# Attention units of one pair of heads over half a batch instead of over a whole batch, with the scores negated, in a fused attention and two-layer feed-forward kernel

## The reference

```python
q_d, k_d, v_d = mean of q, k, v over groups of 4 tokens        # 144 pooled tokens
out_up = repeat(softmax_attention(q_d, k_d, v_d), 4)
mask = |pos_i - pos_j| < 4
out_local = softmax(where(mask, scale * q k^T, -1e9)) v        # softmax subtracts the maximum, adds 1e-9 to the sum
x = (out_up + out_local), heads side by side                   # 2304 x 512
h = relu(x @ w_in); g = s * h * h + b; x = g @ w_out           # d_ff 2048
out = ((x @ w_a) * (x @ w_b)) @ w_out2                         # d_ff 1536
```

## Time and profile before

| | us |
|---|---|
| median of 3 runs | 1069.96 (1068.77 to 1071.46) |
| the profiled execution, whole | 1069.81 |
| its span in the trace | 1068.0 |
| PE busy in the span | 1009.2 (94%) |
| DVE, ACT, POOL busy | 442.6, 356.3, 159.4 |
| start of the first matmul of slot 0 and of slot 1 of the first layer | 74.10, 81.21 |
| start of the second layer | 596.06 |

### The profile page before, as it was taken

How to read it: one execution, slowest core, us unless ns; L and a number is a source line. 1 busy time by engine, 2 the same in 40 slices (tenths; PEclk the granted TensorE clock), 3 DMA queues, 4 the chain that set the end, 5 groups by cost and what they waited for, 6 DMA issues and landing times.

```text
span 1068.0 us, 17004 instructions
## 1 busy us (share of the span) xinstructions
PE 1009.2 (94%) x6984; PEld 944.7 (88%) x6984; DVE 442.6 (41%) x800; ACT 356.3 (33%) x791; POOL 159.4 (15%) x126
## 2 busy tenths in 40 slices
PE   5678899999999999999999799999999999999997
PEld 4557889999999999999999699899899898998996
DVE  4768665565555655554345521211211212112111
ACT  3445444444344443344245421211211212212211
POOL 4545343122331223310000000000000000000000
PEclk9659999999999999999999899999999999999999
DMA  7343401121011210201033600010100100100000
GB/s 193 77 124 112 126 20 50 45 68 46 17 52 46 68 46 15 55 13 43 10 111 119 200 1 1 20 40 1 57 3 1 60 1 1 60 1 1 30 2 30
DMA packets 98829, 52.50 MB, mean 49 GB/s; under 512 B 60384, under 2 KB 92768, under 8 KB 98752
## 3 DMA queue, kind: packets, MB, share of 16 engines
q1 hardware_dynamic: 98608, 51.35, 17.3%
q10 hardware_dynamic: 144, 0.07, 0.0%
HBM read 41.97 MB, written 9.44 MB: 48 GB/s over the span
## 4 chain that ended last, share of the span: by engine, by line
PE 85%; DVE 6%; ACT 3%; POOL 3%; issue 2%; DMA 1%; SPq 0%; ACTq 0%; DVEq 0%; POOLq 0%
PE bank L667 28%; PE bank L632 18%; PE bank L617 17%; PE bank L681 13%; PE bank L546 2%; PE bank L493 2%; PE bank L517 2%; PE bank L467 1%; DVE relu L992 1%; POOL sm L1073 1%; PE bank L478 1%; POOL sm L1081 1%; PE bank L538 1%; POOL wx L1088 1%; PE bank L512 1%
## 5 line engine op out<-in xcount | busy, mean ns | idle before, releaser
L667 PE MATMUL bank<-x_hi,wx 128*128 128x384 f32 x1152 | 307.0, 337 | 11.8 <-DVE prod L1051 7.8
L632 PE MATMUL bank<-g_hi,wx 128*128 128x288 f32 x1024 | 234.2, 305 | 1.4 <-DVE o_sb L1004 1.4
L617 PE MATMUL bank<-wx 128*128 128x288 f32 x1536 | 230.7, 299 | 0.4 <-ACT relu L792 0.4
L667 PEld LDWEIGHTS bank<-x_hi,wx 128*128 128x128 f32 x1152 | 210.2, 188 | 17.3 <-issue 14.4
L617 PEld LDWEIGHTS bank<-wx 128*128 128x128 f32 x1536 | 211.8, 190 | 3.4 <-issue 2.8
L667 PE MATMUL bank<-x_lo,wx 128*128 128x384 f32 x576 | 193.5, 336 | 0.0
L632 PEld LDWEIGHTS bank<-g_hi,wx 128*128 128x128 f32 x1024 | 171.9, 189 | 9.5 <-issue 4.2
L1051 DVE TENSOR_TENSOR prod<-bank,a_sb 128x384 f32<-128x384 f32 x72 | 40.1, 558 | 314.5 <-ACT a_sb L854 314.5
L632 PE MATMUL bank<-g_lo,wx 128*128 128x288 f32 x512 | 151.5, 296 | 0.0
L992 DVE SCALAR_TENSOR_TENSOR relu<-relu,s_col 128x288 f32<-128x288 f32 x128 | 81.7, 638 | 166.4 <-ACT relu L792 166.2
L854 ACT ACTIVATE a_sb<-bank 128x384 f32<-128x384 f32 x72 | 35.3, 491 | 303.7 <-PE bank L667 303.7
(11 more groups left out here) (67 smaller groups left out, 821.4 us busy)
## 6 DMA issues: line engine op xcount, KB each, us to landing
nat<-in_q SPq DMA_DIRECT2D x32, 144.0 KB, 2.9
nat<-in_k SPq DMA_DIRECT2D x32, 144.0 KB, 3.2
vnat<-in_v SPq DMA_DIRECT2D x32, 144.0 KB
o_transposed<-o_sb SPq DMA_DIRECT2D x8, 576.0 KB, 3.2
o_raw<-o_transposed SPq DMA_DIRECT2D x6, 768.0 KB, 4.7
out<-y SPq DMA_DIRECT2D x18, 256.0 KB, 2.2
vwin<-in_v SPq DMA_DIRECT2D x32, 120.0 KB
raw<-in_moe_w_a SPq DMA_DIRECT2D x12, 256.0 KB, 3.1
```

The costliest lines, as they stand in the source:

```text
L617: mm = nc.tensor.matmul(HB[:, 0:HALF], wi(w, kd, f), xs(x, c % 2)[:, kd], start=(kd == 0 and j == 0), stop=(kd == KD - 1 and j == 2))
L632: mm = nc.tensor.matmul(ACC[o][:, 0:HALF], wo(w, f, o), g[:, slot % GB, :], start=(f == 0 and j == 0), stop=(f == F1 - 1 and j == 2))
L667: mm = nc.tensor.matmul(dst[:, 0:CH2], wab(w, f, j * KD + kd), x[:, kd, :], start=(kd == 0 and m == 0), stop=(kd == KD - 1 and m == 2))
```

## The change

The work is no longer cut by pair-batches but by units: one pair of heads over half a batch (288 tokens), 32 in all, in the order of the chunks of the first layer. A unit takes 4 slots. What needs the whole batch, which is k (turned and pooled) and the pooled v, is made by the unit of the first half of a batch (`leads(u)`) and kept for the second half. The boot now holds four units (first half of batch 0), each with a set of buffers of its own, and 28 units run beside the first layer. Within a unit:

- q and k are turned in ticks -5 and -4, that is in the gap between the scores and the turned probabilities of the unit before;
- pooled and local scores come together in tick 0, in banks 0, 1 and 2; the pooled and local probabilities are turned together in tick 6, the values come together in tick 7;
- q is scaled by -1/8, so scores have the other sign; the mask is subtracted, minima take the place of maxima, and the minimum goes into exp as a bias (scale -1). GpSimd's `subtract` goes; exp of the local scores is six instructions of 102 columns in place of one of 612;
- the 1e-9 is a column of the array that is summed, so one small addition goes;
- the pooled values are scaled by ScalarE (`take_up`, tick 8) and the sum of both (`take_values`, tick 8) is one VectorE instruction for each unit; `xf` has two buffers;
- 4 blocks of the first layer are split in the boot instead of 6, and from the seventh block on the second layer's are split behind each of its first six steps, none ahead of `take_acc`.

The first loads of k and q are shared by two DMA queues.

```diff
-POOLED, LOCAL0, LOCAL1 = 0, 1, 2
-JOBS = 3
-NP = PAIRS * B
-BOOT_SKEW = 6
-BOOT_END = 11
-BOOT_TICKS = BOOT_SKEW * (PAIRS - 1) + BOOT_END + 1
-BOOT_BLOCK_TICKS = (10, 14, 18, 22, 25, 28)
+NU = PAIRS * NCH
+SETS = PAIRS
+PER_UNIT = 2 * F1 // PAIRS
+LEAD = 3
+BOOT_SKEW = 6
+BOOT_TICKS = 34
+BOOT_BLOCK_TICKS = (-14, -9, -5, -3)
+EARLY2 = 6
...
+        def bank_before(u):
+
+            return max(u - 1, 0) if u <= PAIRS else u
+
+        def at_tick(g, boot_tick, tick):
+
+
+            first = [u for u in range(PAIRS) if BOOT_SKEW * u - BOOT_TICKS + boot_tick == g]
+            return first + [u for u in range(PAIRS, NU) if PER_UNIT * (u - PAIRS) - LEAD + tick == g]
...
+            def scores(u):
+                _, h, p = place(u)
+                at = base(u)
+                pe.wait_ge(kp_ready, pair(u) + 1)
+                pe.wait_ge(qp_ready, u + 1)
+                past(pe, ptl_taken, bank_before(u))
+                past(pe, o_taken, bank_before(u))
...
+                pooled_scores(0).then_inc(sp_half, 1)
+                for w in range(GW):
+                    for e in (1, 0):
+                        mm = local_scores(e, w)
+                mm.then_inc(sl_ready, 1)
+                pe.wait_ge(sp_half, u + 1)
+                pooled_scores(1).then_inc(sp_ready, 1)
...
+            def attention(g):
+                for u in at_tick(g, 12, 7):
+                    values(u)
+                for u in at_tick(g, 0, -5):
+                    if leads(u):
+                        turn_k(u)
+                for u in at_tick(g, 1, -4):
+                    turn_q(u)
+                for u in at_tick(g, 3, 0):
+                    scores(u)
+                for u in at_tick(g, 11, 6):
+                    turn_pooled(u)
+                for u in at_tick(g, 10, 6):
+                    turn_local(u)
...
+            def exp_local(u):
+                act.wait_ge(mnl_ready, u + 1)
+                for j in range(2 * GW):
+                    x = kits[kit(u)]["sml"][:, j, 0:WK]
+                    done = nc.scalar.activation(x, x, ACT.Exp, bias=mnl(u)[:, j:j + 1], scale=-1.0)
+                done.then_inc(el_ready, 1)
...
+            def take_up(u):
+                act.wait_ge(o_ready, u + 1)
+                past(act, o_taken, before(u))
+                nc.scalar.activation(kits[kit(u)]["up"][:], bank[:, base(u) + 2, HALF:HALF + GH], ACT.Copy,
+                                     scale=1.0 / POOL).then_inc(up_taken, 1)
...
             for slot in range(SLOTS):
                 c, f = divmod(slot, F1)
-                n, at = PAIRS + slot // 8, 2 * (slot % 8)
-                attention(n, at)
-                if slot % (2 * F1) in (1, 2, 3, 4):
-                    split_x_hi(c + 1, f - 1)
+                attention(2 * slot)
                 if f == 2 and c > 0:
                     take_acc(c - 1)
                 take_relu(slot)
-                attention(n, at + 1)
+                attention(2 * slot + 1)
...
-            for f in range(6, 9):
-                split_w2_hi(f)
             take_acc(NCH - 1)
...
+            def take_values(u):
+                dve.wait_ge(up_taken, u + 1)
+                past(dve, x_hi, u - 1)
+                past(dve, x_lo, u - 1)
+                dst = xf[:, u % 2, :].rearrange("p (g r) -> p g r", r=POOL)
+                src = bank[:, base(u) + 2, 0:HALF].rearrange("p (g r) -> p g r", r=POOL)
+                add = kits[kit(u)]["up"][:].unsqueeze(2).to_broadcast([P, GH, POOL])
+                nc.vector.tensor_tensor(dst, src, add, ALU.add).then_inc(o_taken, 1)
...
+            def attention(g):
+                for u in at_tick(g, 14, 8):
+                    take_values(u)
+                for u in at_tick(g, 15, 9):
+                    split_x_lo(u)
...
+                for u in at_tick(g, 4, 0):
+                    minima(u)
...
-            def subtract(n, kind):
-                pool.wait_ge(mx_ready, job(n, kind))
-                x = sm_flat(n, kind).rearrange("p (j c) -> p j c", c=WK)
-                m = mx(n, kind).unsqueeze(2).to_broadcast([WQ, 2 * GW, WK])
-                nc.gpsimd.tensor_tensor(x, x, m, ALU.subtract).then_inc(sub_ready, 1)
```

More of the change, by code:

```diff
@@ L306, in pt_bank, with place, leads, pair @@
-        def pt_bank(n):
-            return 4 * kit(n) + 2 if alone(n) else 1
-        def o_bank(n, kind):
-            return 4 * kit(n) + (1 if kind == LOCAL0 else 0) if alone(n) else 0
-        def boot_tick(at, tick_of):
-            return [p for p in range(PAIRS) if at - BOOT_SKEW * p == tick_of]
+        def place(u):
+            return u // (2 * PAIRS), u // PAIRS % 2, u % PAIRS
+        def leads(u):
+            return place(u)[1] == 0
+        def pair(u):
+            i, _, p = place(u)
+            return PAIRS * i + p
@@ L457, in _ @@
         def _(pe):
-            def turn(n, t):
-                if t == 0:
-                    pe.wait_ge(nat_in[kit(n)], 64 * uses(n))
-                    past(pe, o_taken, job(before(n), LOCAL1))
-                    past(pe, pt_taken, job(before(n), LOCAL1))
-                if t == 3 and not alone(n):
-                    pe.wait_ge(turn_taken, 4 * n + 1)
-                for u in range(GW):
-                    mm = nc.tensor.transpose(bank[:, turn_bank(n, t), u * WQ:(u + 1) * WQ],
-                                             nat(n)[:, t // 2, GW * (t % 2) + u, :], ident[0:WQ, 0:WQ])
-                mm.then_inc(turn_ready, 1)
@@ new lines, in turn_local @@
+            def turn_local(u):
+                pe.wait_ge(pl_done, u + 1)
+                if not alone(u) and u + 1 < NU:
+                    pe.wait_ge(q_taken, u + 2)
+                for e in range(2):
+                    for w in range(GW):
+                        mm = nc.tensor.transpose(bank[0:WK, base(u) + e, w * WQ:(w + 1) * WQ],
+                                                 kits[kit(u)]["sml"][:, GW * e + w, 0:WK], ident[0:WQ, 0:WQ])
+                mm.then_inc(ptl_ready, 1)
@@ L1036, in _ @@
                         split_w2_lo(f // 2 - 2)
-            for f in range(6, 9):
-                split_w2_lo(f)
             take_acc(NCH - 1)
@@ L1124 @@
+            for g in range(-BOOT_TICKS, 0):
+                attention(g)
+                if g in BOOT_BLOCK_TICKS and BOOT_BLOCK_TICKS.index(g) % 2 == 1:
+                    split_w_lo(BOOT_BLOCK_TICKS.index(g))
+            for slot in range(SLOTS):
+                c, f = divmod(slot, F1)
+                attention(2 * slot)
+                attention(2 * slot + 1)
+                if c == 0 and f + BOOT_BLOCKS < F1 and f % 2 == 1:
+                    split_w_lo(f + BOOT_BLOCKS)
 _INS = ['q', 'k', 'v', 'moe_w_in', 'moe_w_out', 'moe_s', 'moe_b', 'moe2_w_a', 'moe2_w_b', 'moe2_w_out']
```

946 lines of the change are left out of this document (386 added, 560 removed).

## The result

The changed kernel takes 1099.89 us (median of 4 runs, 1096.15 to 1102.33), the kernel before in the same series 1070.71 us. The ratio is 1.0269, with a 95% interval of 1.0233 to 1.0305: slower by 2.7%. The forecast was 1099 us. The profiled execution took 1097.56 us, 1095.8 of them its span; the forecast was a span of 1097.

The account below looks back on a forecast made before the run. PE was taken as the bound, busy 1009.2 of 1068.0 us. Terms -15.8 + 13.6 + 0 + 39.2 - 6.7 - 4 = +26.3, plus 3 for the clock, gave 1099 us; range 1080 to 1117 for 8 of 10.

Parts of the forecast that it names:

- Part 4: First layer: PE's scores wait for relu, square and take_values of the unit before, 27 x 1.45 = +39.2 us.
- The condition under which it would have been 2.4 us: Unit boundaries: the new wait would be 2.4 us wherever GpSimd works beside square, 1.45 elsewhere; the sum took 1.45.
- adds nothing: New wait: take_up, about 0.25 us on ACT behind relu, is done before take_values starts, so costs nothing.
- Part 3: ACT: six exps of 102 columns for one of 612, taken as 1.5 us, covered by PE's pace, cost 0.
- the rival: First layer: the exps do come in the way, making the next relu late; +14 us, 1113 us; chance 10%.
- The rest, early waits: Chunk 0 of the first layer: four early waits fewer, -4 us (bounds -8 and +6).
- Part 1: Boot: four units instead of four pair-batches, slot 1 at 65.4 us instead of 81.2, -15.8 us (bounds -28 and 0).
- Part 2: First layer: attention moved out of the boot adds PE work, +13.6 us (bounds +8 and +20).
- the clock: First layer: two stretches at 1.2 GHz behind the 27 new waits, +3 us.
- Part 5: Start of second layer: four splits leave the path ahead of the first product; shorter wait -5.3, clock -1.4, together -6.7 us.
- The clock falling at each wait: Rival, first layer: half clock behind each of 27 new waits, 46 us more, 1145 us; chance 5%.
- The hidden wait: Rival: the new wait is hidden and the shorter boot decides; sum -12.9, 1057 us, faster; chance 5%.

Follow-up runs that it names:

- run 1: Changed kernel with take_up and take_values one tick earlier (7 instead of 8), ahead of relu and square: 1058.76 us, ratio 0.9894 to the kernel before.
- run 3: Kernel before the change, with the taking of the pooled values moved from tick 8 to 9, behind square: 1085.54 us, ratio 1.0151.
- Run 2: Changed kernel with only take_values at tick 7, ahead of square; take_up stays behind relu: 1090.22 us, ratio 1.0198 to the kernel before.
- run 4: Changed kernel with one exp of 612 columns for six, leaving out the minimum's subtraction in the local softmax: 1085.92 us, ratio 1.0149 to the kernel before.
- run 7: As run 1, with local probabilities turned and copied ahead of the pooled ones in tick 6: 1045.38 us, ratio 0.9780 to the kernel before.
- run 5: Changed kernel with three second-layer weight splits (blocks 6, 7, 8) put back ahead of take_acc: 1102.40 us, ratio 1.0305 to the kernel before.
- run 6: As run 5, with the fourth split also back, ahead of a_sb and prod in the step: 1109.26 us, ratio 1.0369 to the kernel before.
- run 10: Changed kernel with take_values and the next unit's minima behind split_g_lo on DVE, beside the first layer: 1159.98 us, ratio 1.0849 to the kernel before.

## Why the prediction was right, and where its steps failed

The time was right and its main term too. Other terms were off, in directions that cancelled.

**Part 4, the new wait: right.** Predicted 27 x 1.45 = 39.2 us, found 27 times 1.51, 40.9. The place (L498 for L858), the count and the links of the chain are as told; run 1 takes the wait away and gains 41.1, run 3 makes it in the old kernel. The condition under which it would have been 2.4 us, square stretched beside GpSimd, did not come: at all the unit boundaries square takes 0.52. Run 2 adds what the step had left as "adds nothing": `take_up` decides as soon as square is out of the way.

**Part 3, the exps at nothing: the step that failed.** I sized six exps at 1.5 us (found 1.73) and looked for cover in the tightest slot, but asked only whether relu comes in time. It does. Who else stands behind the exps on ACT I didn't follow: the pooled exps, the weights on DVE, GpSimd's multiplication and the turn of the pooled probabilities. Run 4 prices it at 14.0 us by the medians and 11.4 by the profiled spans, near the figure that the rival had, but by another way than the relu of that rival: PE's wait for the turn (12.6 to 6.1 us), 4.2 us of busy time and 1.5 of boot. The term belonged in the sum. That its absence did no harm is luck: two other terms, boot and busy time, were forecast too high.

**The rest, early waits -4: wrong.** The idle time of the first layer beside the new wait is 52.9 - 40.9 = 12.0 us, that of before 12.2. It is the pooled turn, above all its two waits of 3.0 us in chunk 0. Part of this is part 3 again, seen from PE; with one exp the two waits are still above 2 us (run 4).

**Part 1, the boot: -18.8, predicted -15.8.** The units start at 4.96, 10.53, 22.39 and 32.96 against 5.2, 10.6, 22.8 and 34.1; the period is 10.6 instead of 11.3. The rest, from unit 3 to slot 1, is 29.4 instead of 31.3. The mechanism held, and the sizes were within a microsecond or two.

**Part 2 and the clock: together +12.0 of busy time, predicted 13.6 + 3 = 16.6.** From 62 to 132 us the clock is 0.92, which is 5.6 us; before it was 0.98 over the first 68.8 us of the stage, 1.4 us. So the clock took some 4 us, and the attention moved here some 8 us, the lower bound of part 2, where 13.6 was forecast. The unit periods tell a part of the 5.8 between them. In the changed kernel they are 18.65 and 17.80; less the wait of 1.51 us, that of 0.33 in every second group and four slots of the earlier trace rows, 3.83 a unit are left, 7.7 a pair-batch, where I had taken 7.9 in the earlier trace rows: some 3 us over 14 pair-batches. Where the other 3 are I did not settle. In run 7 the periods are 16.60 and 16.06, which is 7.2 a pair-batch. The clock loss, forecast at 3, was put in the wrong place, and that its size came near is luck: there was none behind the 24 waits from 135.94 us on, and all of it lay in the first slots, where identical code loses 6 us more in another execution (run 5).

**Part 5, -6.7, found -6.8, for another reason.** Of the four splits that leave the path, three cost next to nothing where they were (run 5: 0.2 us of wait). With the fourth, which waited for its DMA, the wait was back (run 6: 5.57 us). I had counted splits where the question was which one waits.

**The rivals.** The clock falling at each wait was given 5% at 1145; with waits of 1.51 us it did not happen, with 2.63 us it did behind 18 of 24 (run 10). Its condition was the length, as the two idle times of the earlier trace rows had hinted, though at 2.63 us the length alone did not decide: 6 of the 24 were followed by full clock. The Trainium skill (TensorE: Matmul & The Clock Gate, "HAM oscillation — how this bites in real kernels") tells of a kernel in which a wait for DMA of about 3 to 5 us in every tile lets the clock fall each time. The changed kernel's waits, at 1.51 us, are half of that or less, so this account gave no reason to expect 1145; run 10 shows the fall at 2.63 us already, and no run here has such regular waits of 3 to 5. The hidden wait, with a faster kernel at 1057, is what run 1 built: 1058.76.

Adding the terms as measured: -18.8 (boot), +12.0 (busy time, clock in it), +40.9 (new wait), -0.2 (other idle time), -6.8 (second layer), and 0.6 between the edge of the window and the second layer's start: +27.7. The forecast's were -15.8, +16.6, +39.2, -4, -6.7: +29.3. It came within 0.1% because 7.6 too much (boot 3.0, busy time 4.6) stood against 5.5 too little (new wait 1.7, other idle time 3.8). The main term was foreseen; this closeness was luck.

## What to carry to other kernels

When a buffer changes hands between two units inside one slot, look at what stands ahead of the releasing instruction on every engine that touches it: here a place half a slot earlier on two engines turned 2.7% slower into 1.1% faster, and a second swap, of two turns, into 2.2% faster. To cost added work at nothing, follow each consumer queued behind it to the engine that sets the end, not only the most obvious one. When a stall ends in a product behind several pieces of work, ask which of them waits itself, before counting them all.

## What the runs showed of the hardware that was not expected

- TensorE's clock bore regular idle times of one length and not of another: the waits of 1.51 us, one per 17.8 to 18.65 us, left 1.00 from 135.94 to 554.78 us; waits of 2.63 us at the same places gave 0.94 over the same work, with half clock behind 18 of 24. Regular waits of a length in between were not tried.
- Identical code took 59.62 and 65.73 us of PE's time for the same 496 matmuls in the first slots (run 5). The whole kernel's executions, 1096.15 to 1102.33 us, lie as far apart. A gain of a few microseconds near a boot needs windows over the same work to be believed.
- The granted clock in the trace was 0.98 over a boot in which a turn of six matmuls took 1.22 us instead of 0.66.
- Square takes 0.52 us alone and 1.37 beside GpSimd's multiplication. In chunk 0, beside a GpSimd split, it took 1.77, and a `TENSOR_SCALAR` of 72x2 took 1.17 us instead of 0.15:

```profile
82.53 2.42 POOL L1000 TENSOR_TENSOR wx<-stage,wx 128x1024 fp32r<-128x1024 f32 x1 [10.06 <-ACT wx L729]
...
83.50 1.77 DVE L903 SCALAR_TENSOR_TENSOR relu<-relu,s_col 128x288 f32<-128x288 f32 x1 [0.52 <-ACT relu L744]
...
84.91 1.42 POOL L985 TENSOR_TENSOR sml<-sml,stat 96x612 f32<-96x612 f32 x1
...
85.19 1.17 DVE L840 TENSOR_SCALAR stat<-stat 72x2 f32<-72x2 f32 x1
```

- One exp of 96x102 takes 0.37 us, as one of 144 columns did, but six in a row take 1.73 us from the first start to the last end, since they overlap; one of 96x612 had taken 0.71. One microsecond more on an engine that is busy 35% of the time, 28 times beside the first layer and 4 in the boot, still cost the kernel 14.0 us by the medians and 11.4 by the profiled spans (run 4).

```profile
L679 ACT ACTIVATE sml<-sml,stat 96x102 f32<-96x102 f32 x192 | 55.2, 370 | 4.1 <-DVE stat L831 4.1
```
